# A fused attention and feed-forward kernel on one core: the second Z of step 0 goes into the first tile, one gram eviction to VectorE, the sums of squares become two products and the last outputs go out by parts

## The reference

```
delta-rule attention: B, H, S, D = 4, 8, 768, 48
  for t: y[t] = q[t] @ state;  state += beta[t] * outer(k_n[t], v[t] - k_n[t] @ state)
x = y as (3072 tokens, 384)
first network:  h = x @ w_in (384 x 2048);  g = 0 | (h+1)^2/4 | h by h <= -1, in between, h >= 1;  x2 = g @ w_out
second network: xn = x2 / sqrt(mean(x2^2) + 1e-6) * rms_g
                out = (silu(xn @ w_gate) * (xn @ w_val)) @ w_out2        (w_gate, w_val: 384 x 1536)
```

## Time and profile before

| | us |
|---|---|
| median of 3 runs (1058.16 to 1059.16) | 1059.01 |
| the profiled execution's own time | 1059.34 |
| its span, first to last instruction | 1057.4 |
| busy in the span: TensorE | 1033.4 |
| VectorE | 535.6 |
| ScalarE | 467.9 |

### The profile page before, as it was taken

The page is one execution under the profiler, slowest core; times in us unless marked ns, Lnnn a source line. Parts: engine busy times, 40 slices in busy tenths (PEclk is TensorE's granted clock), DMA queues, the critical chain, the costliest instruction groups (busy, mean ns, idle before and its releaser), DMA issues.

```text
span 1057.4 us, 25018 instructions
## 1 busy us (share of the span) xinstructions
PE 1033.4 (98%) x11128; PEld 852.4 (81%) x11128; DVE 535.6 (51%) x1003; ACT 467.9 (44%) x841; POOL 9.6 (1%) x20
## 2 busy tenths in 40 slices
PE   8899899999999999999999999999999999999996
PEld 4489788777777777777778888888888888888885
DVE  6768469657747837843356434333234333333322
ACT  6755744654663484464466443232232232232211
POOL 1000000000000000000000000000000000000000
PEclk9999999999999999999999999999999999999999
DMA  9407004102300500120111220200200100100101
GB/s 265 130 4 150 3 4 121 32 3 61 91 3 22 130 3 3 44 108 2 61 61 60 90 91 1 60 1 3 58 1 31 31 1 1 30 1 1 30 1 30
DMA packets 19034, 48.09 MB, mean 45 GB/s; under 512 B 2448, under 2 KB 9232, under 8 KB 17872
## 3 DMA queue, kind: packets, MB, share of 16 engines
q1 hardware_dynamic: 18800, 46.11, 16.2%
q10 hardware_dynamic: 128, 0.39, 0.2%
HBM read 37.06 MB, written 9.44 MB: 44 GB/s over the span
## 4 chain that ended last, share of the span: by engine, by line
PE 91%; ACT 3%; DVE 2%; issue 2%; DMA 1%; DVEq 0%; SPq 0%; ACTq 0%
PE bank L722 21%; PE hps L1286 18%; PE acc L1301 18%; PE acc L741 10%; PE hps L722 7%; PE hps L741 4%; PE acc L1325 1%; PE bank L1245 1%; PE bank L1179 1%; PE bank L1224 1%; PE bank L1231 1%; PE bank L1208 1%; PE bank L1258 1%; DMA stage<-w_in 1%; PE bank L1169 1%
## 5 line engine op out<-in xcount | busy, mean ns | idle before, releaser
L639 ACT ACTIVATE g<-bank 128x512 f32<-128x512 f32 x72 | 43.1, 598 | 257.3 <-PE bank L722 142.7
L1286 PE MATMUL hps<-xh,w1h 128*128 128x512 f32 (+1 forms) x336 | 129.8, 386 | 3.1 <-DVE g L1117 2.3
L1301 PE MATMUL acc<-g1h,w2h 128*128 128x512 f32 (+1 forms) x336 | 127.0, 378 | 0.3 <-ACT x2s L962 0.3
L1286 PE MATMUL hps<-xl,w1h 128*128 128x512 f32 (+1 forms) x336 | 122.3, 364 | 0.0
L1286 PE MATMUL hps<-xh,w1l 128*128 128x512 f32 (+1 forms) x336 | 122.0, 363 | 0.0
L1301 PE MATMUL acc<-g1l,w2h 128*128 128x512 f32 (+1 forms) x336 | 122.0, 363 | 0.0
L1301 PE MATMUL acc<-g1h,w2l 128*128 128x512 f32 (+1 forms) x336 | 121.8, 362 | 0.0
L954 ACT ACTIVATE g1h<-g 128x512 fp32r<-128x512 f32 (+1 forms) x112 | 63.9, 571 | 128.6 <-DVE g L1117 117.0
L1125 DVE TENSOR_TENSOR g1l<-g,g1h 128x512 fp32r<-128x512 f32 (+1 forms) x112 | 68.5, 611 | 92.0 <-ACT g1h L954 91.6
L1117 DVE SCALAR_TENSOR_TENSOR g<-hps,g 128x512 f32<-128x512 f32 (+1 forms) x112 | 68.1, 608 | 59.4 <-ACT g L948 59.4
L945 ACT ACTIVATE g<-hps,half_c 128x512 f32<-128x512 f32 (+1 forms) x112 | 69.7, 622 | 45.7 <-PE hps L1286 45.0
(11 more groups left out here) (191 smaller groups left out, 2029.2 us busy)
## 6 DMA issues: line engine op xcount, KB each, us to landing
kqT<-kq SPq DMA_DIRECT2D x22, 384.0 KB, 6.8
v_in<-v SPq DMA_DIRECT2D x6, 768.0 KB, 4.2
k_in<-k SPq DMA_DIRECT2D x6, 768.0 KB, 6.0
x2d<-x2s SPq DMA_DIRECT2D x18, 256.0 KB, 5.6
x2t<-x2d SPq DMA_DIRECT2D x6, 768.0 KB, 6.0
y<-y_t SPq DMA_DIRECT2D x48, 96.0 KB, 2.2
stage<-w_in SPq DMA_DIRECT2D x4, 768.0 KB, 8.7
stage<-w_gate SPq DMA_DIRECT2D x3, 768.0 KB, 4.4
```

Source lines behind the costliest of these rows:

```text
L639: act.activation(silu[:, f % 2, :], gps[f % 2][:, :], ACT.Silu).then_inc(e_silu, 1)
L1286: last = pe.matmul(hps[f % 2][:, 0:WIDTH[n]], wt[:, kk, P * f:P * f + P], xx[:, kk, COLS[n]], start=(kk == 0 and e == 0), stop=(kk == KD - ...
L1301: last = pe.matmul(acc[j][:, 0:WIDTH[n]], wt[:, f, P * j:P * j + P], gg[:, f % 2, 0:WIDTH[n]], start=(f == 0 and e == 0), stop=(f == NF1 - ...
```

## The change

It does these things:

- The eviction of the fourth quarter of step 1's gram (GE 1,3) goes from ScalarE to VectorE, and its place from beside the inversion to behind U's and PU's outputs of the first half.
- Z, its eviction and `up` of step 0's second half go from the first stretch into the first tile, at places 3, 3 and 4; KU goes from 6 to 5, X from 3 to 6, and XB now takes half of X's eviction there too.
- Banks of step 0 are dealt anew; a bank of `acc` is waited for by the low piece that used it last, not by all 24.
- `ones` becomes float32r, written by ScalarE and not by GpSimd.
- The folded squares are split into a high part (ScalarE, `sumhi`) and a low part (VectorE, `sumlo`), and the sum is two float32r products.
- For the last slice of the last tile TensorE does the eight products with the high part first and then the four with the low part, with a signal for each bank; VectorE copies banks 0 and 2, ScalarE 1 and 3; SyncE issues four of the eight stores, ScalarE the other four.

```diff
@@ first_body
-            ev += {13: [("GK", 1, 0)], 14: [("GE", 1, 0)], 15: [("GE", 1, 1)], 16: [("GK", 1, 1)], 17: [("GE", 1, 2)], 18: [("GE", 1, 3)],
+            ev += {13: [("GK", 1, 0)], 14: [("GE", 1, 0)], 15: [("GE", 1, 1)], 16: [("GK", 1, 1)], 17: [("GE", 1, 2)],
...
-    out += [("X", 0, 0), ("vnh", 0, 0), ("XB", 0, 0), ("GQE", 0, 0)] + piece(22) + low(22) + [("U", 0, 0), ("Z", 0, 1), ("ZE", 0, 1)]
-    out += [("vnh", 0, 1), ("PU", 0, 0)] + piece(23) + [("XT", 0, n) for n in range(KD)] + low(23)
-    out += [("XE", 0, n) for n in range(KD)] + [("up", 0, 1)]
+    out += [("X", 0, 0), ("vnh", 0, 0), ("XB", 0, 0), ("GQE", 0, 0)] + piece(22) + low(22) + [("U", 0, 0), ("vnh", 0, 1), ("PU", 0, 0)]
+    out += piece(23) + [("GE", 1, 3)] + [("XT", 0, n) for n in range(KD)] + low(23) + [("XE", 0, n) for n in range(KD)]
@@ second_half
-    return [(3, ("X", 0, 1)), (3, ("XD", 0, 1)), (6, ("KU", 0, 0)), (9, ("KS", 0, 1)), ...
+    return [(3, ("Z", 0, 1)), (3, ("ZE", 0, 1)), (4, ("up", 0, 1)), (5, ("KU", 0, 0)), (6, ("X", 0, 1)), (6, ("XD", 0, 1)), (6, ("XB", 0, 1)),
+            (9, ("KS", 0, 1)), ...
@@ FIRST
-         ("Z", 0, 0): (3,), ("X", 0, 0): (4,), ("U", 0, 0): (2, 3), ("Z", 0, 1): (4,), ("PU", 0, 0): (1, 0),
-         ("XT", 0, 0): (3,), ("XT", 0, 1): (2,), ("XT", 0, 2): (0,), ("X", 0, 1): (1,), ("KU", 0, 0): (2, 0)}
+         ("Z", 0, 0): (3,), ("X", 0, 0): (4,), ("U", 0, 0): (3, 5), ("PU", 0, 0): (1, 0), ("XT", 0, 0): (3,),
+         ("XT", 0, 1): (4,), ("XT", 0, 2): (0,), ("Z", 0, 1): (2,), ("KU", 0, 0): (1, 0), ("X", 0, 1): (2,)}
@@ last_round, second_network
-              ("gl", n, 1): [("square", 0, 2), ("fold", 0, 0)],
+              ("gl", n, 1): [("square", 0, 2), ("fold", 0, 0), ("sumhi", 0, 0)],
...
-    norms = {2: ["square"], 3: ["fold"], 4: ["sums", "root"], ...
+    norms = {2: ["square"], 3: ["fold", "sumhi", "sumlo"], 4: ["sums", "root"], ...
@@ second_scalar
+                elif kind == "sumhi":
+                    act.wait_ge(e_fold, n + 1)
+                    act.activation(sumh[:, :], x2sq[:, 0, :], ACT.Copy).then_inc(e_fh, 1)
...
+                elif kind == "out" and n == NSTEP - 1:
+                    act.wait_ge(e_out, n * N_OUT)
+                    for j in range(1, NT4, 2):
+                        act.wait_ge(e_ylast, j + 1)
+                        act.activation(y_t[:, j, :], yps[j][:, 0:DM], ACT.Copy).then_inc(e_ya, 1)
+                    for j in range(NT4):
+                        last_out_ready(act, j)
+                        y_store(act, n, j, 1)
@@ second_vector
+                elif kind == "sumlo":
+                    dve.wait_ge(e_fh, n + 1)
+                    dve.tensor_tensor(suml[:, :], x2sq[:, 0, :], sumh[:, :].bitcast(F32), ALU.subtract).then_inc(e_fl, 1)
@@ second_tensor
-                    pe.wait_ge(e_fold, n + 1)
+                    pe.wait_ge(e_fl, n + 1)
...
-                    pe.matmul(sums_of(n)[:, :], ones[:, :], x2sq[:, 0, :], start=True, stop=True).then_inc(e_ss, 1)
+                    pe.matmul(sums_of(n)[:, :], ones[:, :], sumh[:, :], start=True, stop=False)
+                    pe.matmul(sums_of(n)[:, :], ones[:, :], suml[:, :], start=False, stop=True).then_inc(e_ss, 1)
...
+                    if (n, f) == (NSTEP - 1, NF2 - 1):
+                        pe.wait_ge(e_prh, NSTEP * NF2)
+                        for j in range(NT4):
+                            for wt in (woh, wol):
+                                pe.matmul(yps[j][:, 0:DM], prh[:, f % 2, P * j:P * j + P], wt[:, f, :], start=False, stop=False)
+                        pe.wait_ge(e_prl, NSTEP * NF2)
+                        for j in range(NT4):
+                            pe.matmul(yps[j][:, 0:DM], prl[:, f % 2, P * j:P * j + P], woh[:, f, :], start=False, stop=True)                                .then_inc(e_ylast, 1)
+                        return
@@ banks_free
-                                pe.wait_ge(s_wl, PIECES * NCHUNK)
+                                pe.wait_ge(s_wl, NPIECE - KD + (b - (NPSUM - KD)) + 1)
```

More of the change, by code:

```diff
@@ L280, in second_network @@
 def second_network():
-    norms = {2: ["square"], 3: ["fold"], 4: ["sums", "root"], 6: ["invert"], 7: ["invert"], 8: ["scale"], 9: ["hi"], 10: ["lo"]}
+    norms = {2: ["square"], 3: ["fold", "sumhi", "sumlo"], 4: ["sums", "root"], 6: ["invert"], 7: ["invert"], 8: ["scale"], 9: ["hi"], 10: ["lo"]}
     parts = {0: (15, 17), 1: (17, 19), 2: (19, 20), 3: (20, 21), 4: (21, 22), 5: (22, 24), 6: (24, 26), 7: (26, 27)}
@@ L324, in build @@
         half_c = sb("half_c", [P, 1])
-        ones = sb("ones", [P, P])
+        ones = sb("ones", [P, P], F32R)
         eps_c = sb("eps_c", [P, 1])
@@ L577, in load_x2, with y_store, last_out_ready @@
                 sp.dma_start(x2t[n % 2][:, :, :], x2d[n, :, :, :]).then_inc(e_x[n % 2], 16)
+            def y_store(eng, n, j, m):
+                hf, bp = j // BP, j % BP
+                eng.dma_start(y_rows[bp ^ m, m, n * STEP + hf * C:n * STEP + hf * C + C, :], y_t[C * m:C * m + C, j, :])\
+                    .then_inc(e_out, 16)
+            def last_out_ready(eng, j):
+                if j % 2:
+                    eng.wait_ge(e_ya, j // 2 + 1)
+                else:
+                    eng.wait_ge(e_yc, (NSTEP - 1) * NT4 + j // 2 + 1)
             def second_sync(sp):
@@ L684, in second_vector @@
                     dve.tensor_tensor(prl[:, f % 2, :], pr[:, f % 2, :], prh[:, f % 2, :].bitcast(F32), ALU.subtract).then_inc(e_prl, 1)
+                elif kind == "out" and n == NSTEP - 1:
+                    dve.wait_ge(e_out, n * N_OUT)
+                    for j in range(0, NT4, 2):
+                        dve.wait_ge(e_ylast, j + 1)
+                        dve.tensor_copy(y_t[:, j, :], yps[j][:, 0:DM]).then_inc(e_yc, 1)
                 elif kind == "out":
@@ L848, in _ @@
                     pool.memset(eps_c[:, :], 1e-6).then_inc(s_const, 1)
-                    pool.memset(ones[:, :], 1.0).then_inc(s_const, 1)
                     pool.memset(state[:, :, :], 0.0).then_inc(s_const, 1)
@@ L862, in attention @@
                         kind, c, hf = u
-                        if kind == "GE":
+                        if kind == "GE" and hf < NQ - 1:
                             u = ("GK", c, hf // NQH)
-                            j = hf % NQH
+                            own, j = 1 if u in by_vector else NQH, hf % NQH
                             act.wait_ge(p_gk, half(c, hf // NQH))
@@ L872, in attention @@
                                                       bank_of(u, j)[r, :].rearrange("p (i t) -> p i t", t=C)[:, :, 0:BLK], ACT.Copy)
-                            last.then_inc(s_gk, 1)
+                            last.then_inc(s_gk, NQH // own)
                         elif kind == "GK" and c != 1:
@@ L876, in attention @@
                             own = 1 if u in by_vector else NQH
-                            done = own * hf if c == 0 else NQ * (c - 1) + NQH * hf + HALVES
+                            done = own * hf if c == 0 else NQ * (c - 2) + NQH * hf + HALVES + NQ - 1
                             for j in range(own):
@@ L911, in attention @@
                             act.wait_ge(s_up, half(c, hf))
-                            for m in range(MEM if c or hf else 1):
+                            for m in range(MEM if c else 1):
                                 for e in range(MEM):
@@ L978, in _ @@
                     act.activation(nident[:, :], ident[:, :], ACT.Copy, scale=-1.0).then_inc(s_neg, 1)
+                    act.activation(ones[:, :], half_c[:, 0:1].to_broadcast([P, P]), ACT.Copy, scale=2.0)
                     for plan in PLANS:
@@ L1061, in attention @@
                                               ALU.mult).then_inc(s_vn, 1)
-                        elif (kind, c) == ("GK", 0):
-                            dve.wait_ge(p_gk, half(c, q))
-                            mine = slice(NPAIR * q + H, NPAIR * q + 2 * H)
-                            dve.tensor_copy(gram[0][:, mine, :], bank_of(u, 1)[:, :].rearrange("p (i t) -> p i t", t=C)).then_inc(s_gf2, 1)
-                            dve.wait_ge(s_gf2, q + 1)
+                        elif u[:2] == ("GK", 0) or u == ("GE", 1, NQ - 1):
+                            n = HALVES - 1 if c else q
+                            u = ("GK", c, n)
+                            dve.wait_ge(p_gk, half(c, n))
+                            mine = slice(NPAIR * n + H, NPAIR * n + 2 * H)
+                            dve.tensor_copy(gram[c][:, mine, :], bank_of(u, 1)[:, :].rearrange("p (i t) -> p i t", t=C)).then_inc(s_gf2, 1)
+                            dve.wait_ge(s_gf2, by_vector[u][1])
                             for r in UPPER:
-                                last = dve.tensor_copy(gram[0][r, mine, BLK:C],
+                                last = dve.tensor_copy(gram[c][r, mine, BLK:C],
                                                        bank_of(u, 1)[r, :].rearrange("p (i t) -> p i t", t=C)[:, :, 0:BLK])
```

(2 more changed lines are left out.)

28 lines of the change are left out of this document (17 added, 11 removed).

## The result

The kernel after takes 1050.72 us (median of 4 runs, 1049.63 to 1052.6), the kernel before on the same chip 1059.09 (4 runs, 1058.16 to 1061.16): 8.4 us less, a ratio of 0.992 with a 95% interval of 0.99 to 0.9941. On another chip it was 1050.48 (4 runs, 1049.91 to 1051.15) against 1059.74 (10 runs), 0.9913 (0.99 to 0.9926). Predicted were 1050.2 and 1048.4 to 1053.4.

A forecast was written before the change was run, and what follows sets the result against it. TensorE, busy 98% of the span, was taken as the bound, with gains at its waits, start and end. Start -3.8, sums -2.3 and last outputs -2.7 gave -8.8 us: 1050.2 us predicted, range 1048.4 to 1053.4.

The forecast's parts named there:

- X: First stretch: moving one gram eviction off ScalarE starts X 1.1 us earlier, bounds 0.65 to 1.25.
- The stop and the low clock: First stretch: without the second Z, PU loses its 1.8 us instruction stop, ends 3.55 earlier; network starts 3.7 earlier.
- the 0.67 us that the first `h` was to get back: First tile: nine matmuls of `h` take 1.27 us instead of 1.94, as the clock is no longer low.
- Rival 1: Start: the stop only moves, so the start gains about 1.2 us; total -6.2, 1052.8 us, chance 0.17.
- VectorE's extra work: First tile: XB adds 0.86 us to VectorE, absorbed by idle time; bounds 0 and +0.9 for TensorE.
- Sums: Sums of squares in six tiles: 0.40 us less each, -2.3 us in all, bounds -1.5 and -2.6.
- Tail: Last outputs: earlier products, shared copies and two store queues give -2.7 us, bounds -0.9 and -3.2.
- a floor of 3.6 us of DMA work: Last stores: 16 DMA engines need 3.6 us from 1050.3 on, so the end can't come before 1053.9.
- Rival 2: Last stores: ScalarE's queue gains nothing, landing late; last part -0.9 only, total -7.0, 1052.0 us, chance 0.12.
- Rivals 3 and 4: Low clock held from the first tile, 1062 us, chance 0.05; start and sums gain nothing, 1058.5 us, chance 0.04.
- rival 3: First tile: short waits hold the clock at 0.5 for 22 us, costing 11.7; 1062 us, chance 0.05.

The follow-up runs named there:

- the shifted kernel: Kernel before with one of four warming products left out and 64 small products added on TensorE at the start: 1064.51 us, one run.
- sums alone: Kernel before with only the sums of squares changed to two float32r products: 1057.73 us, ratio 0.9987.
- tail alone: Kernel before with only the last outputs changed (products by parts, copies on two engines, stores on two queues): 1056.21 us, ratio 0.9971.
- z stays: Kernel after with the second Z, its eviction and `up` back ahead of PU, X and KU placed as before: 1054.02 us, ratio 0.9944.
- the shifted kernel after: Kernel after with 26 small products (104 instructions) added between the first two grams: 1054.08 us, one run.
- the start alone: Kernel before with only the edits to the first stretch and first tile: 1055.84 us, ratio 0.9968.

## Why the prediction was right, point by point

**X.** Predicted 1.1 us earlier, seen 1.4 behind the inversion (44.11 - 14.74 against 42.59 - 14.64). All of ScalarE's 1.4 us came back here, over the 1.25 I had as bound: the queue was solid and nothing else was due. Where the inverse comes later, less does.

**The stop and the low clock.** Predicted: PU runs through and ends at 48.1, `h` at 50.9; seen 47.98 and 50.70. The step "a block border that fell on PU's last matmul falls elsewhere" held: the border at number 1473 was PU's last weight load, and the count over all traces shows that the stops go with the borders. That the clock falls because of the stop isn't shown: the shifted kernel had 1.71 us of stop and a clock of 1.00 behind it, and the kernel after, run again, 1.8 us of idle time at 120 without a fall. What is seen is that four of the four profiled executions with the stop in PU had the clock at 0.5 for 3.4 to 6.8 us, in three of them from within the stop on (sums alone from 51.33, tail alone 51.02, z stays 49.65); the stop of 1.91 us in GK(1,1) had it too, from 35.89; and of the seven with this start none fell between 40 and 60. So it is open whether the 0.67 us that the first `h` was to get back, and did, come from the missing stop; luck can have a part in them. One term was put too low: between U's copy and PU stand 0.37 us, not 0.05 (0.37 to 0.56 in the seven executions). Border 1217, which stood ahead of the second Z before, now stands at PU's waits; in the shifted kernel after, with no border there, it is 0.24. So most of it is the handover, and the rest the border. X's extra 0.3 paid for it.

**Rival 1** (the stop moves) happened in part: 0.61 us in the second X, where the prediction allowed 1.0 in its sum. It is border 1729, and its stop differs between executions: 0.06 us in the start alone, 0.34 to 0.37 in three, 0.61 to 0.63 in the other three. The first tile's stretch from `h` to GQ(0,1) is 9.35 us against 9.58, -0.2, where -0.1 was predicted. VectorE's extra work (XB, the eviction) reached TensorE nowhere that the traces show: GQ(0,1) to tile 1 takes 36.08 to 36.24 us in the seven executions and 36.00 before, but 36.02 in z stays, where VectorE has the same extra work. The rule of the Trainium skill ("Runtime: NRT & Kernel Launch", section "Instruction fetch mechanics"), that crossing a border is mostly hidden, agrees with this case in the second network, where no border shows a stop of 0.5 us, and doesn't for runs of small matmuls, where TensorE stood up to 1.91 us at one.

**Sums.** Predicted -2.3, seen -1.9 to -2.0. The size of one was to be 0.40 and is 0.35 to 0.38 (0.39 to 0.44 for tile 0's). What was mis-sized most is tile 1: "2.3, since in tile 1 the square root also waits" took 0.1 off, the root took 0.3, as moving it ahead shows.

**Tail.** Predicted -2.7, seen -3.1 to -3.2, the far bound. The mis-sized term is the end: from the low part's start to the end of the span were predicted 7.6 us and seen 7.55 (1040.23 to 1047.78), but the kernel before took 10.7 (1046.67 to 1057.36) and not 10.3, since I ended it with the last store's median landing. That 7.6 was met is luck: it rested on a floor of 3.6 us of DMA work that wasn't there (see the end). Without the floor the terms were 3.08 to ScalarE's first issue, 1.85 to its last and 2.2 to landing, 7.13; they came as 2.54, 2.07 and 2.59, with 0.35 from there to the end of the span. ScalarE's queue starts at 1042.77, before its copies end, beside its own second copy: the first bank it stores is VectorE's; and its four issues take 2.67, not 2.4. Rival 2 is out: its stores land after 2.5 us (SyncE's 2.2 to 2.4). The Trainium skill ("DMA: Bandwidth & Descriptors", "Issuing engines are not separate DMA queues") calls what a second issuing engine saves usually small; here it was 1.9 us.

**Rivals 3 and 4** did not come. The low clock of rival 3 does show up elsewhere (10 us at 123 us with the eviction on ScalarE), for some 3 us and not 12.

## What to carry to other kernels

Count TensorE's instructions, its waits included, as well as its time: where a chain of "issue" stands inside a run of small matmuls, see whether it goes with the instruction count, and put large products between such runs before shortening them. At the end of a kernel, look at what is serial (a split, copies, a queue's issues) and give each half of it to an idle engine. When one product is shortened, read which wait ends last behind it; here a root that had been hidden took most of one tile's gain.

## What was not expected of the hardware

- TensorE's stops for instructions end 2.2 to 2.9 us behind a 16 KB instruction transfer (2.5 to 2.8 for those at 51.40, 57.74, 35.49 and 56.04), and all stand at the same place of a count by 256 that has the waits in it.
- The eight last stores kept the 16 DMA engines busy for 0.68 x 5.30 = 3.6 us from one queue, and for 0.51 x 5.40 = 2.8 us from two, for the same 0.79 MB. The one queue in the kernel after gives 33.0% of 11 us, 3.6 again. So the busy share from one queue was no fixed amount of work, and the floor of 3.6 us that the prediction took from it was too high.
- The low clock comes in some executions and not in others of the same kernel: the executions of the kernel before have mean clocks of 0.993 to 0.999 and times of 1058.65 to 1061.68 on one chip. What decides it is open.
